# Attention and two feed-forward blocks on one core: loads, pooling, slots and the activation of tile 0 rearranged

## The reference, cut to what matters

```
out_d     = softmax(scale * mean4(q) @ mean4(k).T) @ mean4(v)    # positions pooled by 4
out_local = softmax(scale * q @ k.T where |i - j| < 4) @ v
x = repeat(out_d, 4) + out_local                                 # 2304 x 512
h = x @ w_in                                                     # 512 -> 2048
g = where(h > 0, h, exp(min(h, 0)) - 1)                          # the activation of block one
y = g @ w_out                                                    # 2048 -> 512
z = (silu(y @ w_gate) * (y @ w_val)) @ w_out2                    # 512 -> 1536 -> 512
```

## Time and profile before

| | us |
|---|---|
| median of three runs | 1000.27 (1000.21 to 1001.07) |
| the profiled execution, its own time | 999.19 |
| its span, first to last instruction | 997.3 |
| TensorE busy | 985.8 (99%) |
| VectorE busy | 455.7 (46%) |
| ScalarE busy | 341.0 (34%) |
| GpSimd busy | 115.0 (12%) |
| TensorE idle behind VectorE's weight subtraction (L616) | 2.8, four times |

### The profile page before, as it was taken

How to read it: one execution, slowest core, us unless ns; L and a number is a source line. 1 busy time by engine, 2 the same in 40 slices (tenths; PEclk the granted TensorE clock), 3 DMA queues, 4 the chain that set the end, 5 groups by cost and what they waited for, 6 DMA issues and landing times.

```text
span 997.3 us, 17826 instructions
## 1 busy us (share of the span) xinstructions
PE 985.8 (99%) x7040; PEld 912.5 (91%) x7040; DVE 455.7 (46%) x1151; ACT 341.0 (34%) x953; POOL 115.0 (12%) x138
## 2 busy tenths in 40 slices
PE   8899999999999999999999999999999999999998
PEld 5889999999999999999999888888888888889997
DVE  7888755556555565564343332223222322322222
ACT  5565544444435344443346321212121221212112
POOL 7204510023000000000057500000000000000000
PEclk9999999999999999999999999999999999999999
DMA  8544521124102111110434300200020001001000
GB/s 241 184 123 106 104 52 43 45 60 100 33 26 77 42 38 33 58 30 1 154 120 131 116 1 1 76 1 1 1 77 1 1 29 47 1 1 39 1 1 37
DMA packets 45666, 55.68 MB, mean 56 GB/s; under 512 B 6504, under 2 KB 33992, under 8 KB 45584
## 3 DMA queue, kind: packets, MB, share of 16 engines
q1 hardware_dynamic: 38128, 50.61, 16.5%
q0 software_dynamic: 6816, 3.55, 2.6%
q10 hardware_dynamic: 640, 0.39, 0.2%
HBM read 45.08 MB, written 9.44 MB: 55 GB/s over the span
## 4 chain that ended last, share of the span: by engine, by line
PE 95%; DVE 2%; ACT 2%; DMA 1%; issue 0%; ACTq 0%; POOL 0%; DVEq 0%; POOLq 0%
PE bank L455 29%; PE bank L457 28%; PE bank L456 28%; PE bank L419 2%; PE bank L386 2%; PE bank L404 1%; PE bank L441 1%; PE bank L395 1%; ACT weights L785 1%; DMA q_first<-qT 1%; DVE weights L616 1%; PE bank L429 0%; ACT prob L746 0%; DVE g_sb L641 0%; ACTq L360 0%
## 5 line engine op out<-in xcount | busy, mean ns | idle before, releaser
L455 PE MATMUL bank<-x_hl,weights 128*128 128x464 f32 (+3 forms) x928 | 325.8, 351 | 4.0 <-DVE weights L616 2.8
L457 PE MATMUL bank<-x_hl,weights 128*128 128x464 f32 (+3 forms) x928 | 322.0, 347 | 0.0
L456 PE MATMUL bank<-x_hl,weights 128*128 128x464 f32 (+3 forms) x928 | 321.9, 347 | 0.0
L455 PEld LDWEIGHTS bank<-x_hl,weights 128*128 128x128 f32 x928 | 175.5, 189 | 15.3 <-DVE weights L616 3.9
L456 PEld LDWEIGHTS bank<-x_hl,weights 128*128 128x128 f32 x928 | 175.6, 189 | 10.2
L457 PEld LDWEIGHTS bank<-x_hl,weights 128*128 128x128 f32 x928 | 175.5, 189 | 10.3
L455 PE MATMUL bank<-g_hl,weights 128*128 128x384 f32 (+1 forms) x448 | 147.7, 330 | 0.0
L457 PE MATMUL bank<-g_hl,weights 128*128 128x384 f32 (+1 forms) x448 | 143.3, 320 | 0.0
L456 PE MATMUL bank<-g_hl,weights 128*128 128x384 f32 (+1 forms) x448 | 143.2, 320 | 0.0
L659 DVE TENSOR_TENSOR u_sb<-bank,u_sb 128x464 f32<-128x464 f32 (+1 forms) x60 | 38.3, 638 | 202.3 <-ACT u_sb L807 202.3
L807 ACT ACTIVATE u_sb<-bank 128x464 f32<-128x464 f32 (+1 forms) x60 | 33.3, 555 | 196.4 <-PE bank L457 196.4
(11 more groups left out here) (96 smaller groups left out, 1062.5 us busy)
## 6 DMA issues: line engine op xcount, KB each, us to landing
landing<-w SPq DMA_DIRECT2D x44, 256.0 KB, 4.0
v_win<-v_windows SPq DMA_DIRECT2D x46, 105.0 KB
q_sb<-qT SPq DMA_DIRECT2D x88, 48.0 KB, 2.3
k_sb<-kT SPq DMA_DIRECT2D x14, 288.0 KB, 3.7
yT_scratch<-y_sb SPq DMA_DIRECT2D x20, 192.0 KB, 2.0
y_raw<-yT_scratch SPq DMA_DIRECT2D x4, 928.0 KB, 5.3
outT<-out_sb SPq DMA_DIRECT2D x16, 232.0 KB, 2.3
landing<-wg SPq DMA_DIRECT2D x12, 256.0 KB, 2.9
```

The source lines that it names most:

```text
L455: nc.tensor.matmul(out, w_hi, x_hi, start=first, stop=False)
L456: nc.tensor.matmul(out, w_hi, x_lo, start=False, stop=False)
L457: return nc.tensor.matmul(out, w_lo, x_hi, start=False, stop=last)
```

## The change

It makes eight edits, all in what runs in the first 140 us:

1. The q transfers of the prologue are divided: the first half of each goes on SP's queue ahead of its k, the second on ScalarE's.
2. k of unit 1 is pooled by GpSimd, not VectorE.
3. v is summed in the order 0, 1, 2, 3; unit 0 now waits for GpSimd's sum (12 products) and unit 1 takes raw v (48 products).
4. Fillers 2 and 5 instead of 4 and 3; the transposes of unit 1 go ahead of the outputs of unit 0.
5. ScalarE's and VectorE's order of copies and weight pieces in the prologue.
6. Slot 0 (scores of unit 4) goes ahead of the hidden product of step 2.
7. In tile 0 the activation is relu(-h) and exp(-that) on ScalarE, the second waiting for the first, and one VectorE operation, max(e - 1, h).
8. The slots of units 8 to 15: scores at 22, 26, 30, 34, 38, 42, 44, 48 instead of 20, 24, ..., 48; the other pieces move with them.

```diff
-ORDER_V = [1, 0, 2, 3]
-SUMMED_BY_PRODUCT = (0, 2, 3)
+SUMMED_BY_PRODUCT = (1, 2, 3)
-    S_SLOT[_u] = 20 + 4 * (_u - 2 * PAIRS)
+    S_SLOT[_u] = (22, 26, 30, 34, 38, 42, 44, 48)[_u - 2 * PAIRS]
     NORM_SLOT[_u], T_SLOT[_u], O_SLOT[_u] = S_SLOT[_u] + 3, S_SLOT[_u] + 5, S_SLOT[_u] + 8
...
-            pe_filler(pe, 4)
+            pe_filler(pe, 2)
             pe_transposes(pe, 0)
-            pe_filler(pe, 3)
+            pe_filler(pe, 5)
+            pe_transposes(pe, 1)
             pe_outputs(pe, 0)
-            pe_transposes(pe, 1)
             pe_transposes(pe, 2)
...
+            pe_slot(pe, 0)
             for s in range(STEPS):
                 if s + 2 < STEPS:
                     pe_hidden(pe, s + 2)
-                pe_slot(pe, 2 * s)
+                if s > 0:
+                    pe_slot(pe, 2 * s)
...
             dve.wait_ge(e_done, s + 1)
+            if s < NF1:
+                nc.vector.scalar_tensor_tensor(g, g, -1.0, hid[s % 2][:, 0:n], ALU.add, ALU.max).then_inc(g_done, 1)
+                return
...
+            if s < NF1:
+                nc.scalar.activation(g_sb[:, s % 2, 0:n], hid[s % 2][:, 0:n], ACT.Relu, scale=-1.0).then_inc(r_done, 1)
+                act.wait_ge(r_done, s + 1)
+                nc.scalar.activation(g_sb[:, s % 2, 0:n], g_sb[:, s % 2, 0:n], ACT.Exp, scale=-1.0).then_inc(e_done, 1)
+                return
...
             for u in range(PROLOGUE):
-                load_q(act, u)
+                load_q(act, u, 1)
...
-            for u in range(2, PROLOGUE):
+            for u in range(1, PROLOGUE):
                 pool_pool_k(pool, u)
-            for i in range(PAIRS):
-                pool_pool_v(pool, i)
+            for p in range(PAIRS):
+                pool_pool_v(pool, p)
...
             for u in range(PROLOGUE):
+                load_q(sp, u, 0)
                 load_k(sp, u)
```

More of the change, by code:

```diff
@@ L262, in build @@
         hid_done, acc_done = sem("hid_done"), sem("acc_done")
+        r_done = sem("r_done")
         e_done, t_done, g_done = sem("e_done"), sem("t_done"), sem("g_done")
@@ L351, in by_token, with load_q @@
             return x.rearrange("p (j r) -> p j r", r=POOL)
-        def load_q(eng, u):
+        def load_q(eng, u, half):
             a, p, j = batch_of(u), pair_of(u), third_of(u)
             done = qk_first_loaded[u - 2] if 2 <= u < PROLOGUE else qk_loaded[u % 2]
-            for half in range(2):
-                rows = slice(DH * half, DH * half + DH)
-                eng.dma_start(q_home(u)[rows, half, :], qT[a, p, rows, j * GROUP:(j + 1) * GROUP]).then_inc(done, 16)
+            rows = slice(DH * half, DH * half + DH)
+            eng.dma_start(q_home(u)[rows, half, :], qT[a, p, rows, j * GROUP:(j + 1) * GROUP]).then_inc(done, 16)
         def load_k(eng, u):
@@ L388, in pe_scores @@
             pe.wait_ge(q_pooled, u + 1)
-            if a == 0 and p >= 2:
-                pe.wait_ge(k_late_pooled, p - 1)
+            if a == 0 and p > 0:
+                pe.wait_ge(k_late_pooled, p)
             elif j == 0:
-                pe.wait_ge(k_pooled, a * PAIRS + p + 1 if a == 0 else a * PAIRS + p - 1)
+                pe.wait_ge(k_pooled, 1 if a == 0 else (a - 1) * PAIRS + p + 2)
             for half in range(2):
@@ L433, in pe_outputs @@
             if a == 0:
-                pe.wait_ge(v_pooled, ORDER_V.index(p) + 1)
+                pe.wait_ge(v_pooled, p + 1)
             else:
@@ L638, in dve_elu @@
             dve.wait_ge(e_done, s + 1)
+            if s < NF1:
+                nc.vector.scalar_tensor_tensor(g, g, -1.0, hid[s % 2][:, 0:n], ALU.add, ALU.max).then_inc(g_done, 1)
+                return
             nc.vector.tensor_scalar(g, g, 1.0, -1.0, ALU.min, ALU.add).then_inc(t_done, 1)
-            dve.wait_ge(t_done, s + 1)
+            dve.wait_ge(t_done, s + 1 - NF1)
             nc.vector.scalar_tensor_tensor(g, hid[s % 2][:, 0:n], 0.0, g, ALU.max, ALU.add).then_inc(g_done, 1)
@@ L684, in _ @@
             dve_pool_q(dve, 1)
-            dve_pool_k(dve, 1)
             dve.wait_ge(masks_set, 6)
@@ L698, in _ @@
             dve_x_low(dve, 0)
+            dve_weight_low(dve, 0)
             dve_output(dve, 1)
-            dve_weight_low(dve, 0)
             dve_x_low(dve, 1)
@@ L839, in _ @@
             act_exps(act, 3)
+            act_copies(act, 1)
             act_weight_a(act, 0)
-            act_copies(act, 1)
             act_copies(act, 2)
             act_x_high(act, 0)
+            act_weight_a(act, 1)
             act_copies(act, 3)
             act_x_high(act, 1)
-            act_weight_a(act, 1)
             act_weight_a(act, 2)
@@ L891, in pool_pool_k @@
             wait_qk(pool, u)
-            wait(pool, k_late_pooled, u - 2)
+            wait(pool, k_late_pooled, u - 1)
             x = by_token(k_home(u))
@@ L895, in pool_pool_k, with pool_pool_v @@
                 nc.gpsimd.tensor_tensor(k_halves[:, :, r], x[:, :, r], x[:, :, r + 2], ALU.add).then_inc(k_half_sums, 1)
-            pool.wait_ge(k_half_sums, 2 * (u - 1))
+            pool.wait_ge(k_half_sums, 2 * u)
             nc.gpsimd.tensor_tensor(k_pool[:, pair_of(u), :], k_halves[:, :, 0], k_halves[:, :, 1],
                                     ALU.add).then_inc(k_late_pooled, 1)
-        def pool_pool_v(pool, i):
-            p = ORDER_V[i]
+        def pool_pool_v(pool, p):
             pool.wait_ge(v_raw_loaded[p], 64)
@@ L911, in pool_pool_v @@
             pool.wait_ge(zero_rows_set, 3)
-            pool.wait_ge(v_half_sums, 2 * TILES * (i + 1))
+            pool.wait_ge(v_half_sums, 2 * TILES * (p + 1))
             for c in range(TILES):
@@ L962, in load_qk @@
             sp.wait_ge(scores_done, u - 3 if u < 6 else u - 1)
-            load_q(sp, u)
+            load_q(sp, u, 0)
+            load_q(sp, u, 1)
             load_k(sp, u)
@@ L983, in load_piece_a @@
             if n >= ALIASED:
-                sp.wait_ge(k_late_pooled, 2)
+                sp.wait_ge(k_late_pooled, 3)
                 sp.wait_ge(v_pooled, PAIRS)
```

## The result

Over 20 executions of each kernel the changed one takes 1005.0 us (median; 1001.12 to 1009.16), the one before 1000.03 (998.38 to 1002.29). The ratio is 1.0053, 95% interval 1.0041 to 1.0065: slower by 0.5%, where 998.6 was forecast. The profiled execution took 1007.06, its span is 1005.2; before 999.19 and 997.3.

The account below looks back on a forecast made before the run. Tile 0's strict-order loop between ScalarE and VectorE was taken as the bound before 67 us, TensorE being busy 985.8 of 997.3. Terms -1.3 - 0.5 - 0.3 + 0.4 = -1.7 us gave 998.6 us; forecast's own range 997.6 to 999.5, overall 995.8 to 1000.4.

Parts of the forecast that it names:

- the slots' price of nothing for units 8 to 10: Slots behind 67 us: units 8 to 10 leave VectorE two slots later, where TensorE doesn't wait; cost 0.
- so I keep it: First hidden products: the 1.2 GHz stretch, costing about 1.7 us, stays unchanged; elsewhere -1, or +1.7 with a second one.
- Term 4: At about 120 us: unit 14's scores at slot 44 wait for their copy, TensorE idle, +0.4 us (0.3 to 0.5).
- Term 1: Prologue, edits 1 to 5: block one begins at 22.9 instead of 24.19 us, -1.3 us (bounds -1.7 and -0.1).
- rival B: Prologue: v of unit 0, or GpSimd, is late; prologue gives 0.1 to 0.5, total -0.5, 999.8 us; chance 0.13.
- Terms 2 and 3: Start of block one, edits 6 and 7, -0.5 us; tile 0's loop of ScalarE and VectorE, edit 7, -0.3 us.
- Rival C: Tile 0: ScalarE's exponential starts much later after its relu; at 0.6 us extra, +2.2, 1002.5 us; chance 0.05.
- rival A: Tile 0: TensorE's waits vanish altogether, VectorE's queue being the limit; 994.6, median 995.7 us; chance 0.17.
- term 3: Tile 0's loop: five waited-for activations longer, +0.45, against VectorE operations saved, -0.75; -0.3 us, +1.3 at the far end.
- a rule against it: Tile 0: the Trainium skill puts relu on VectorE; by it sixteen activations cost 0.06 each, the edit +1 us.

Follow-up runs that it names:

- B: The kernel before, without any of the eight edits; median 1000.03 us over 20 executions, 999.1 to 1000.5 in the follow-up sessions.
- A: The changed kernel with all eight edits, against the kernel before; median 1005.0 us over 20 executions, ratio 1.0053.
- "first half" kernel: The kernel before with units 8 and 9 alone two slots later (scores at 22, 26), units 10 to 15 where they were; 1006.89 us, ratio 1.0073.

## Why the prediction was wrong

**The failed step is the slots' price of nothing for units 8 to 10.** It read: "Units 8 to 10 leave VectorE two slots later, behind 67 us, where TensorE doesn't wait: 0". The trace of before indeed has no wait there, but a place without waits is one where the present order has enough distance; it says nothing of what happens when pieces move. The step looked at VectorE, which the pieces leave, and not at ScalarE, where they arrive, and it did not ask what ScalarE does once per tile: four copies of 0.97 us that the next tile's first accumulation needs. Of a moved slot the exponentials, the transposed copy and their order against `act_y` had to be listed. With them the estimate would have been 1.4 us from the start of the copies to TensorE's (90.52 to 91.94), of which the copies take 0.97, against 2 to 3 us of new work and waiting ahead of them. The runs show it: putting the copies first takes the border from 20.0 and 18.5 us back to B's 14.6, 3.9 us off the median of edit 8 alone, and about 2.3 off A at clock 1.000 (1001.12, a single execution, to 998.8).

**Of the clock, "so I keep it" failed too.** It was bounded at +1.7, a second fall of the same length. In the profiled execution the clock was low 3.4 us longer at the start, 3.4 behind the new wait, and 3.4 at 52 us, which mostly replaced waits. At clock 1.000 A costs some 2 us more than B (one execution); the median costs 5. The rest goes with the clock. How much of it edit 8's wait brings is shown for single executions alone: 1.7 us in A, 3.4 with edit 8 alone. That all five executions of edit 8 alone are at 0.993 to 0.995 doesn't show it, since the kernel with the copies first is mostly as low without the wait.

**Term 4, +0.4, was right for what it named:** one wait ahead of unit 14's scores, for L757:

```profile
119.30 0.59 PE L384 MATMUL bank<-k_sb,q_sb 128*64 128x70 f32 x12 [0.25 <-issue]
```

```profile
118.72 0.48 ACT L757 ACTIVATE probT<-bank 118x384 f32<-118x384 f32 x1
```

The copy ends at 119.20, the scores start at 119.30; the products of the step before take 1.82 instead of 1.43 us to the next start, 0.39. What it left out is some 1.3 us for four groups of small products more.

**Term 1, -1.3: its links failed.** The first was unit 0 at 4.4 us. TensorE no longer waits for it (scores at 5.47, behind the fillers), but VectorE, which needs the same loads, starts on it at 5.50, where before it was 5.68. The next was GpSimd: its first pooling begins at 7.74, not 6.3, after 1.47 us of waiting for k (before it waited 2.87 for a q).

```profile
5.50 0.55 DVE L570 TENSOR_REDUCE q_pool<-q_sb 128x96 f32<-128x384 f32 x1 [2.22 <-DMA k_sb<-kT]
...
7.74 0.85 POOL L903 TENSOR_TENSOR k_halves<-k_sb 128x144 f32<-128x144 f32 x2 [1.47 <-DMA k_sb<-kT]
...
12.44 2.72 POOL L917 TENSOR_TENSOR v_raw<-v_raw 48x128 f32<-48x128 f32 x6 [0.31 <-DMA v_raw<-v_rows]
15.29 1.40 POOL L921 TENSOR_TENSOR v_pool<-v_raw 48x128 f32<-48x128 f32 x3
...
16.55 0.51 PE L402 MATMUL bank<-ident,prob_first 128*118 128x128 f32 x3 [0.76 <-DVE prob_first L595]
```

The first v is summed at 16.69, 0.2 us later than in the earlier trace rows, where 15.1 was forecast: rival B. The other lane, normalisation, was as late: unit 1's, put at 14.5, is what TensorE waits 0.76 us for in the last line, until 16.55. Rival B priced a late v at -0.5 to -0.1 for the prologue; edits 1 to 5 alone gave +0.4, with an interval from -1.4 to +2.1, which settles neither. In A block one began at 26.60 instead of 24.19, with one 0.59 us gap and the clock at 0.50 from 24.5, which makes the last 48 small products 1.0 us longer than in the earlier trace rows:

```profile
22.80 0.90 PE L427 MATMUL bank<-probT_first,v_raw 48*64 48x48 f32 x24 [0.59 <-issue]
...
24.13 2.54 PE L427 MATMUL bank<-probT_first,v_raw 48*64 48x48 f32 x48
26.60 0.53 PE L453 MATMUL bank<-x_hl,weights 128*128 128x192 f32 x1
```

Other kernels with edits 1 to 5 began it at 23.89, 24.46 and 24.85, the one with edits 2 to 5 at 25.74, kernels with the prologue of B at 23.8 to 25.4 and once, behind a gap of 0.9 us of the same kind, at 26.43. So most of A's 2.4 us can't be laid to the edits. What the gap was is not known.

**Terms 2 and 3 stood in their mechanism.** Ahead of the hidden product of step 2 TensorE is idle 0.17 instead of 1.07 us, and the activation runs as worked out:

```profile
32.69 0.33 PE L453 MATMUL bank<-x_hl,weights 128*128 128x192 f32 x1 [0.17 <-DVE g_sb L641]
```

```profile
39.84 0.32 ACT L780 ACTIVATE g_sb<-bank 128x192 f32<-128x192 f32 x1
...
40.18 0.36 ACT L782 ACTIVATE g_sb<-g_sb 128x192 f32<-128x192 f32 x1
...
40.58 0.35 DVE L641 SCALAR_TENSOR_TENSOR g_sb<-g_sb,bank 128x192 f32<-128x192 f32 x1 [1.22 <-ACT g_sb L782]
```

The exponential starts 0.34 us after the relu (0.35 forecast), 0.73 to 0.74 until VectorE; there is no table load. Rival C is false. VectorE waits more and longer, as forecast; against the earlier trace rows, 30 to 68 us:

```profile
DVE g_sb L641 <- ACT g_sb L782: 8.7, 7, 2.5
```

The longest of them, 2.5 us at 32.2, belongs to the slow start. TensorE still waits 3.0 us in four for L616 in the kernel with the copies first, which has no slow start, so rival A is false as well: less work on VectorE did not take these waits away. Together the two terms were put at -0.8; the two edits gave 1.0 by the ratio of the kernel that has them alone, with about 0.2 of it in the loop, where term 3 had 0.3. The relu on ScalarE did not cost the 1 us that the prediction worked out for a rule against it: alone it gave -0.7, with an interval from -1.7 to +0.2.

## What to carry to other kernels

When pieces of work move between slots, list for every engine that they touch what stands behind their new place, and look first for what that engine does only once per tile; an engine order with no wait in it has a distance, and the distance, in us, is what a move spends. A wait of 2 us on an otherwise dense TensorE is priced with the clock behind it: here its 2.0 us came with 3.4 and 6.8 us at 1.2 GHz in two profiled executions, and taking it away gave back 3.9 by the medians. And an edit of which several parts cancel should be read one part at a time: the prologue, the activation and both edits around it were worth between +0.4 and -1.0 us here, and one line cost 6.4.

## What the runs showed of the hardware

- **The clock fell 0.9 and 1.0 us after an idle stretch of 2.0 us had ended**, for 3.4 us in one kernel and 6.8 in another with the same stretch, and 3.4 us at 1.2 GHz cost 1.7 us. With the stretch taken out no fall came there in either. The 2.7 us ahead of 86.59 in the "first half" kernel were followed by none in the execution that was profiled (clock 1.000); its five others had 0.986 to 0.995, but no trace says where. So a fall followed in two of three profiled executions: the wait alone doesn't decide it. The fall at 51.8 us in A began 1.8 us after a wait of 1.3 us for L616; the waits of 1.2 us in B were followed by none.
- **The times of one binary go with its granted clock**: A from 1001.12 at 1.000 to 1009.16 at 0.992, B over 4 us. It isn't all: at 0.992 alone A took 1006.8 to 1009.2. Two kernels are best compared at equal clock beside their medians.
- **Splitting a group of small float32 products in two, with large ones between, cost 0.2 to 0.35 us** without any idle time, seen as longer start-to-start times of the neighbours: 1.40 to 1.49 us for twelve products instead of 1.34. Joining ten groups gave nothing back.
- **Half as many q transfers per queue did not clearly bring the k behind them earlier**: 7.0 to 7.7 us in four kernels with, 7.5 in the one without, one execution each.
